# Local attention ahead of two dense layers: one TensorE product per head on 64 rows, a PSUM bank per head

## What is computed

```python
chunk, left_ctx, right_ctx = (32, 16, 8)          # B, H, S, D = 4, 8, 768, 64; 8 memory keys per head
for c in range(S // chunk):
    k_full = concat([mem_k, k[:, :, l_start:r_end]]); v_full = likewise
    scores = (q_c @ k_full.T) / 8;  a = softmax(scores);  out[:, :, c] = a @ v_full
x = out as (3072 tokens, 512)
h = x @ w_in                     # 512 -> 2048
x = (h * cos(h)) @ w_out         # 2048 -> 512
h = max(x @ w1, x @ w2, x @ w3)  # 512 -> 768
return h @ w_out2                # 768 -> 512
```

## Time and profile before

| what | us |
|---|---|
| median of 3 runs | 1005.51 |
| the three runs | 1004.49, 2384.58, 1005.51 |
| the profiled execution, its time | 1003.52 |
| its span (first to last instruction) | 1001.7 |
| TensorE matmul busy | 962.1 (96%) |
| VectorE, ScalarE, GpSimd busy | 675.9, 516.0, 210.2 |

### The profile page before, as it was taken

How to read it: one execution, slowest core, us unless ns; L and a number is a source line. 1 busy time by engine, 2 the same in 40 slices (tenths; PEclk the granted TensorE clock), 3 DMA queues, 4 the chain that set the end, 5 groups by cost and what they waited for, 6 DMA issues and landing times.

```text
span 1001.7 us, 18402 instructions
## 1 busy us (share of the span) xinstructions
PE 962.1 (96%) x7564; PEld 933.3 (93%) x7564; DVE 675.9 (67%) x926; ACT 516.0 (52%) x689; POOL 210.2 (21%) x231
## 2 busy tenths in 40 slices
PE   5989999999999999999999999999999999999998
PEld 4878889898989899989999999999999999999998
DVE  4355666566665568997998989866736546577761
ACT  1586786867778788333433334543323224444441
POOL 3341111112121212100100000662100000584610
PEclk6799999999999999999999999999999999999999
DMA  9983656574653434443445434432020031324532
GB/s 223 227 212 101 185 149 187 145 201 129 192 165 111 149 131 155 149 145 125 149 145 172 148 106 133 140 120 92 32 95 32 33 127 48 121 95 146 192 116 84
DMA packets 65395, 135.41 MB, mean 135 GB/s; under 512 B 5920, under 2 KB 27424, under 8 KB 65312
## 3 DMA queue, kind: packets, MB, share of 16 engines
q1 hardware_dynamic: 54944, 98.58, 34.2%
q0 software_dynamic: 10368, 35.66, 10.8%
HBM read 87.03 MB, written 47.19 MB: 134 GB/s over the span
## 4 chain that ended last, share of the span: by engine, by line
PE 73%; ACT 10%; DVE 9%; DMA 4%; issue 3%; POOL 1%; SPq 1%; DVEq 0%; ACTq 0%
PE ps L595 23%; PE ps L597 22%; PE ps L596 22%; PE ps L611 2%; DVE work L1178 2%; ACT work L901 2%; PE ps L636 2%; DVE units L1215 2%; ACT work L896 1%; ACT work L903 1%; PE ps L645 1%; DMA early_qk<-qk_in 1%; DVE ssum L1145 1%; ACT work L893 1%; ACT work L872 1%
## 5 line engine op out<-in xcount | busy, mean ns | idle before, releaser
L595 PE MATMUL ps<-units 128*128 128x384 f32 (+1 forms) x1940 | 611.1, 315 | 8.3 <-DVE units L1215 2.0
L597 PE MATMUL ps<-units 128*128 128x384 f32 (+1 forms) x1940 | 602.9, 311 | 0.0
L596 PE MATMUL ps<-units 128*128 128x384 f32 (+1 forms) x1940 | 602.6, 311 | 0.0
L595 PEld LDWEIGHTS ps<-units 128*128 128x128 f32 x1940 | 369.4, 190 | 20.2 <-issue 6.9
L596 PEld LDWEIGHTS ps<-units 128*128 128x128 f32 x1940 | 369.6, 191 | 0.0
L597 PEld LDWEIGHTS ps<-units 128*128 128x128 f32 x1940 | 369.2, 190 | 0.0
L921 ACT CAST units<-work 128x1024 fp32r<-128x1024 f32 x96 | 85.7, 939 | 123.9 <-DVE work L1201 106.6
L1076 ACT COPY work<-ps 128x384 f32<-128x384 f32 (+1 forms) x144 | 63.6, 454 | 146.9 <-PE ps L597 146.8
L1173 DVE SCALAR_TENSOR_TENSOR work<-work 128x768 f32<-128x768 f32 x64 | 62.2, 972 | 71.8 <-ACT work L896 71.8
L1215 DVE TENSOR_TENSOR units<-work,units 128x1024 fp32r<-128x1024 f32 x96 | 102.1, 1105 | 12.2 <-ACT units L921 12.2
L486 POOL DMA_DIRECT2D g_dram<-work x64 | 46.8, 731 | 291.4 <-DVE work L1178 286.7
(11 more groups left out here) (96 smaller groups left out, 845.4 us busy)
## 6 DMA issues: line engine op xcount, KB each, us to landing
g_dram<-work POOLq DMA_DIRECT2D x64, 384.0 KB, 3.3
work<-g_dram SPq DMA_DIRECT2D x48, 512.0 KB, 3.7
work<-qk_in SPq DMA_DIRECT2D x36, 384.0 KB, 5.3
work<-v_in SPq DMA_DIRECT2D x40, 256.0 KB, 5.0
work<-w_in POOLq DMA_DIRECT2D x40, 256.0 KB, 3.6
h_dram<-work SPq DMA_DIRECT2D x24, 384.0 KB, 2.9
work<-h_dram SPq DMA_DIRECT2D x18, 512.0 KB, 3.9
work<-y_dram SPq DMA_DIRECT2D x8, 768.0 KB, 6.5
```

Source lines behind the costliest of these rows:

```text
L595: pe.matmul(o, wh, mh, start=start, stop=False, skip_group_check=onto)
L596: pe.matmul(o, wh, ml, start=False, stop=False, skip_group_check=onto)
L597: return pe.matmul(o, wl, mh, start=False, stop=stop, skip_group_check=onto)
```

## The change

Each head gets a product of its own: stationary 64 rows by 32 columns, moving 64 rows by 64 columns, 32 products for `scores_of` and 32 for `values` in place of 16 and 16. Heads r=0 and r=1 read rows 0 to 63 and 64 to 127 and write two neighbouring banks. The zeros, their memsets and semaphores go; a subtile's keys with queries, and its values, are loaded by one DMA each. Scores (columns 0 to 255) and weighted values (columns 256 to 511) now share banks 4 and 5, turned probabilities are in 6. As two engines must not be in one bank, `values` waits for `shifted` of every scores call that stands ahead of it, and `scores_of` for `o_ready` of the values ahead of it. In block 0 `scores_of(6)` and `shift(6)` move up from f=11 to f=10. The last two pieces are of VectorE's list, block 0.

```diff
-        def scores(n):
-            return ps[:, (4, 0, 2)[n] if n < NSUB else 4, :].rearrange("p (a r k) -> p a r k", a=PAIRS, r=2)
+        def by_head(n, half):
+            if n == 1:
+                banks, at = ps[:, 0:2, :], 0
+            elif n == 2:
+                banks, at = ps[:, 2:4, :], 0
+            else:
+                banks, at = ps[:, 4:6, :], 256 * half if n else 0
+            return banks[:, :, at:at + 256].rearrange("p r (a k) -> p a r k", a=PAIRS)
+        def scores(n):
+            return by_head(n, 0)
...
         def turned(n):
-            return ps[:, (5, 1, 3)[n] if n < NSUB else 5, :].rearrange("p (a t) -> p a t", a=PAIRS)
+            return ps[:, 7 if n == 1 else 6, :].rearrange("p (a t) -> p a t", a=PAIRS)
         def weighted(n):
-            return ps[:, (4, 0, 2)[n] if n < NSUB else 6, :].rearrange("p (a r d) -> p a r d", a=PAIRS, r=2)
+            return by_head(n, 1)
...
-                for r, columns in enumerate((slice(0, KC + SUB), slice(KC, 2 * KC + SUB))):
-                    rows = slice(P // 2 * r, P // 2 * (r + 1))
-                    sp.dma_start(qk_at(n)[rows, :, columns], qk_in[n, rows, :].rearrange("p (a x) -> p a x", a=PAIRS))\
-                      .then_inc(qk_sem(n)[0], 16)
+                sp.dma_start(qk_at(n), qk_in[n, :, :].rearrange("p (a x) -> p a x", a=PAIRS)).then_inc(qk_sem(n)[0], 16)
...
-            clear_values(0)
-            clear_keys(2)
-            clear_values(1)
-            clear_values(2)
...
-            def scores_of(n):
+            def scores_of(n, values_before=0):
                 pe.wait_ge(*qk_sem(n))
-                if n < NSUB:
-                    pe.wait_ge(zeroed[n], 2)
-                else:
+                if n >= NSUB:
                     pe.wait_ge(shifted, n)
-                    pe.wait_ge(o_ready, 1)
+                    pe.wait_ge(o_ready, values_before)
                 pe.sem_inc(tiles_open, 1)
-                q = qk_at(n)
                 for a in range(PAIRS):
                     for c in range(NCH):
                         chunk = slice(CH * c, CH * c + CH)
-                        mm = pe.matmul(scores(n)[chunk, a, :, :], q[:, a, KC + CH * c:KC + CH * c + CH],
-                                       two_parts(q, a, c, KC + SUB), start=True, stop=True)
+                        for r in range(2):
+                            mm = pe.matmul(scores(n)[chunk, a, r, :], queries_in(n, a, r, c), keys_in(n, a, r, c),
+                                           start=True, stop=True)
...
-            def values(n):
+            def values(n, scores_before=0):
                 pe.wait_ge(*v_sem(n))
-                if n < NSUB:
-                    pe.wait_ge(zeroed[3 + n], 2)
-                else:
+                if n >= NSUB:
                     pe.wait_ge(o_ready, n)
+                    pe.wait_ge(shifted, scores_before)
                 pe.wait_ge(pt_copied, n + 1)
...
                 elif f == 6:
                     turn_probs(n + 2)
-                    if later:
-                        scores_of(n + NSUB)
+                    if ahead:
+                        scores_of(n + NSUB, n + 1)
                 elif f == 7:
-                    values(n + 1)
+                    values(n + 1, n + 4 if ahead else SUBS)
...
-                elif f == 9 and later:
-                    scores_of(n + NSUB + 1)
+                elif f == 9 and ahead:
+                    scores_of(n + NSUB + 1, n + 2)
                 elif f == 11:
-                    values(n + 2)
+                    values(n + 2, n + 5 if ahead else SUBS)
...
                             normalise(n + 1)
-                            shift(n + NSUB)
...
                         if f == 10:
+                            shift(n + NSUB)
                             x_low(n)
```

More of the change, by code:

```diff
@@ L104, in program @@
         LEFTOVER = 7 * UCOLS + 6 * 1024
[L105 to L106 removed]
+        early_qk = [plain(f"early_qk{i}", UCOLS * i, PAIRS * (KC + SUB)) for i in range(2)]
+        early_v = [plain(f"early_v{i}", UCOLS * (2 + i), PAIRS * KC) for i in range(2)]
         raw_rows = [plain(f"raw_wi{i}", at, 512 * n) for i, (at, n) in
@@ L314, in load_v @@
                     sp.wait_ge(pv_done, n - 2)
[L315 to L318, removed]
+                sp.dma_start(vals_at(n), v_in[n, :, :]).then_inc(v_sem(n)[0], 16)
             def load_wi(f):
@@ L635, in values @@
                         chunk = slice(CH * c, CH * c + CH)
-                        mm = pe.matmul(weighted(n)[chunk, a, :, :], prob_t(n)[:, a, chunk],
-                                       values_in(n, a, c), start=True, stop=True)
+                        for r in range(2):
+                            mm = pe.matmul(weighted(n)[chunk, a, r, :], prob_t(n)[head_rows(r), a, chunk],
+                                           values_in(n, a, r, c), start=True, stop=True)
                 mm.then_inc(pv_done, 1)
@@ L665, in attend_first @@
                 n = NSUB
[L666 to L671, removed]
+                if f in (0, 2, 4):
+                    scores_of(n + f // 2, n)
                 elif f == 7:
@@ L674, in attend_first @@
                 elif f == 9:
-                    values(n)
+                    values(n, n + 3)
                     turn_probs(n + 1)
@@ L679, in attend_first @@
                     turn_probs(n + 2)
+                    scores_of(n + NSUB, n + 1)
                 elif f == 11:
-                    values(n + 1)
-                    scores_of(n + NSUB)
+                    values(n + 1, n + 4)
                 elif f == 12:
                     turn_out(n + 1)
-                    scores_of(n + NSUB + 1)
+                    scores_of(n + NSUB + 1, n + 2)
                 elif f == 13:
-                    values(n + 2)
+                    values(n + 2, n + 5)
                 elif f == 14:
                     turn_out(n + 2)
-                    scores_of(n + NSUB + 2)
+                    scores_of(n + NSUB + 2, n + 3)
             def attend(t, f):
                 n = NSUB * (t + 1)
-                later = t < NBLK - 2
+                ahead = t < NBLK - 2
                 if f == 1:
```

49 lines of the change are left out of this document (20 added, 29 removed).

## The result

| | before | after |
|---|---|---|
| median, us | 1004.2 (8 runs) | 1011.4 (8 runs, 1008.86 to 1014.69) |
| ratio, 95% interval | | 1.0057 [1.0035, 1.0079] |
| profiled execution: time, span | 1003.52, 1001.7 | 1012.34, 1010.5 |
| TensorE matmul busy | 962.1 | 953.3 |

The change costs 0.6% by this ratio, and the medians are 7.2 us apart: no difference at 2%, but a slower kernel beyond its interval. One of the eight runs before took 2384.58 us, for which nothing here gives a reason, and the ratio leaves it out. The forecast was 1006 in a range of 998 to 1019. The sum of its terms was +1.8 us and the profiled executions differ by 8.8; the table shows that this difference hides two large misses of opposite sign.

The account below looks back on a forecast made before the run. TensorE is busy 96%, but half of each block's chain runs over ScalarE and VectorE, so only five attention groups can give time back. -2.8 - 0.8 - 1.0 + 7.2 - 0.8 = +1.8 us, forecast 1006, range 998 to 1019 with rival 2.

Parts of the forecast that it names:

- The size of a group: Attention groups on TensorE: each saves 0.40 us, within bounds of 0.43 saved and 0.8 lost.
- the supply of instructions: Within each attention group: under 7 ns an instruction, so 128 take at most 0.86 us and maybe half.
- Rival 2: Attention groups: row halves take turns, a group costs what it did, new waits stay; +13.3 us, 1017.5; chance 20%.
- Rival 3: Each of 48 groups: a floor per instruction, slower above about 0.014 us a record; +35 us, 1039; chance 8%.
- The first wait: Blocks 1 to 5, f=7: `values(n+1)` waits for `shift(n+3)`, starting 10.65 us behind `turn_out(n)` for 8.52.
- The second wait: Blocks 1 to 5, f=11: `values(n+2)` waits for `shift(n+4)`, starting 5.89 us behind the scores for 5.39.
- A block: Blocks 1 to 5, `turn_out(n)` to `turn_out(n)`: 46.9 us for 45.5, each 1.4 longer.
- +7.2: Blocks 1 to 5 together: the added waits make each 1.4 us longer, five times.
- The head: Subtiles 0 to 2: -2.8 us, from shorter groups (2.3) and one DMA for two (0.5).
- shorter groups in the head: `scores_of(2)`, `values(1)` and `values(2)` at the lower clock: 0.77 us less each, 2.3 us.
- Block 0: Block 0: -0.8 us from two scores groups ahead of the first evacuation, -1.0 from `turn_out(3)` on.
- Block 6 and the rest: Block 6 has no scores; its two values save 0.8 us, as the third waits anyway.

Follow-up runs that it names:

- E8: Changed kernel with only the first 32 of 64 keys of every score product from subtile 3 on; 1010.61 us in a single run.
- E10: Changed kernel with `sums_w1` later and both shifts earlier on VectorE, the first ahead of `gated`, the second ahead of `turn`; 995.33 us, ratio 0.9913.
- E1: Kernel before with only the new waits and the two moves in block 0, its products, banks and loads kept; 1019.64 us, ratio 1.0147.
- E4: Changed kernel with `sums_w1` moved on VectorE from f=5 to f=8, behind the first `shift` of a block; 1000.04 us, ratio 0.9944.
- E3: Changed kernel, still one DMA a subtile, but each row of keys with queries lands in four pieces of 1.5 KB; 1011.97 us, ratio 1.0061.
- E2: Changed kernel with keys with queries, and values, each loaded by two DMAs of 64 rows instead of one; 1021.81 us, ratio 1.0162.
- E7: Kernel before with only two VectorE moves, `sums_w1` behind f=8 and `shift(n+4)` ahead of `turn` at f=9; 1004.27 us, ratio 1.0004.
- E11: Same kernel as E6, measured again as the base for E10; 996.53 us, ratio 0.992.
- E5: Changed kernel with `shift(n+4)` ahead of `turn` and `gated` of f=9 on VectorE; 1009.96 us, ratio 1.0057.
- E6: Changed kernel with both VectorE moves, `sums_w1` behind f=8 and `shift(n+4)` ahead of `turn` at f=9; 996.73 us, ratio 0.9926.

## Why the forecast came out right, and where its terms did not

- **The size of a group** ("I take 0.40"): nearly twice too much, inside its bounds. It saves 1.01 - 0.79 = 0.22 us, and lasts 0.86 where "about 0.65" was to be seen. The term that failed is the supply of instructions: I had bounded it by "under 7 ns each" and then subtracted 0.03. A cost of 10 ns a record, of one load and one matmul, sets most of the pace (E8). The five groups of TensorE's half give 1.1 us a block, and E10's 44.3 for 45.5 is about that gain with the waits gone.
- **Rival 2, the row halves take turns:** false. At the lower clock `values(1)` lasts 1.18 us (17.19, above) where it lasted 1.94; its last record starts 0.86 behind its first. A wave of 64 columns takes 0.107 at this clock, half of the prediction's 0.21 for 128; sixteen of them in turn would put the last start at 1.6.
- **Rival 3, a floor per instruction:** there is one, but at 10 ns, under the 14 from which it decides. What the Trainium skill gives (TensorE: Matmul & The Clock Gate, Wait — 56ns, not 53.3ns?), 25 ns from start to start, does not hold for products on different tiles: 64 starts lie within 0.64 us.
- **The first wait** ("values(n+1) 10.65"): right in place and cause, and near in size. Measured 10.26, 10.61, 11.82, 11.27 and 10.26. The second and fourth have a memset ahead of the `shift` (0.35 us), the third had a clock drop that cost 1.6 ahead of it, and in the fourth ScalarE had waited 2.16 us for a store to DRAM, a wait that the prediction names in block 0 only. The release takes 0.21 for the 0.25 I used. E1 has it alone, E4 takes it away.
- **The second wait** ("5.89 behind the scores"): 5.86.
- **A block** ("46.9 for 45.5"): 47.7 without a clock drop (block 2), of which 0.5 are groups saving 0.22 for 0.40 (three behind the wait) and 0.36 a longer way to `turn_out` in that block alone. It is there in all nine kernels with the new products and in none of the three with the old; its cause stays open. The other four are 48.5, 48.6, 49.7 and 48.5.
- **The clock** had no term at all, and is most of what separates +7.2 from +15.4; the groups' 0.5 a block are 2.7 more. Four drops in five blocks cost some 1.5 us each, about 6: in block 1, for instance, `turn_out(n+1)` starts 4.50 us behind `values(n+1)` instead of 2.97. I had priced the idle stretch of 2.5 us as only its length. I should have asked what a new idle stretch does to the work behind it. Which drops the new waits cause is shown only in part: three of the four began close behind them and are gone in E4, but drops behind the wait for `turn_out` stay (see the last section).
- **The head** ("one DMA for two mostly saves SyncE issue time: between 0 and 1.0"): this step failed worst. The head has 4.9 us less than forecast in the table's pair, 2.8 on the mean of the traces named under E3. I read the DMA engines as full, and took full for fast: their busy share was 1.0 at half the rate. The Trainium skill has the rule, and I didn't weigh it (SBUF — State Buffer, Door 1: The DMA port swizzle (why `[64,N]` ≈ `[32,N]`)): 64 partitions that are a half of SBUF reach 8 of its 16 DMA ports, for which it gives about 218 GB/s, and 128 reach all, 436. The windows agree, with 220 to 227 and 401. The 2.3 us for shorter groups in the head are not shown by themselves: with the loads in halves (E2) the first wide matmul stands at 32.40, only 0.4 ahead of the kernel before and behind E1 and E7.
- **Block 0** ("-1.8", measured -0.7) is two misses. From the first wide matmul to `turn_out(3)` it took 34.98 us for 36.91, 1.9 less where 0.8 was forecast; the wait for the store to DRAM (9.03) is no longer in the chain. From there to `turn_out(6)` it took 1.2 more where 1.0 less was forecast. `values(4)` starts 6.19 us behind `turn_out(3)` for the forecast 4.7, with no idle time ahead of it, so not for `shift(6)`: TensorE ran at 1.2 GHz from 58.2 to 65.1, across `turn_out(3)` at 60.06, where the drop before the change (62.9 to 66.4) ended ahead of it. The four groups behind add 0.7.
- **Block 6 and the rest** ("-0.8", measured +1.8): inside block 6 the two groups do save, 0.5 us (its last `turn_out` is 20.03 us behind the first for 20.52). Over the kernels with the change this part takes 669.3 us (E3, no clock drop in it) to 673.3 (E11, two). With one drop each, six of them take 671.8 to 672.4, and the three with the old products 670.3 to 671.2, though the layers behind block 6 are untouched. Why is open.

So the total came near by luck: the head's unforeseen 4.9 us stood against the clock's 6 and the groups' missing 0.18 each. The sign was right for its reason, and the waits are shown to be that reason (E1, E4, E7).

## What to carry to other kernels

When buffers are merged so that one engine's next step waits for another engine's list, read in that list what stands ahead of the releaser, and move it in the same change: here one digit (E4) turned a loss of 0.6% into a gain of 0.6%, and two moves into one of 0.8% (three: 0.9%, not told apart). A busy DMA engine is not a fast one: read GB/s beside its share, and load all 128 rows with one transfer (E2: two transfers of 64 rows, 10 us slower). A new idle stretch on TensorE is to be priced with a possible clock drop behind it, not by its length alone.

## What the runs showed of the hardware

- Loads from DRAM to 64 rows move 220 to 227 GB/s with the DMA engines fully busy, to 128 rows 401 (E2 against the changed kernel, the same bytes and packets of about the same size).
- Products on 64 rows and 32 columns run side by side on the row halves (at 1.2 GHz the last of 64 starts 0.86 us behind the first, where sixteen waves in turn would make it 1.6). At 2.4 GHz they start about 10 ns apart with 64 moving columns and 9 ns with 32 (E8), loads of stationary data included.
- Ahead of `values(n+1)` TensorE was idle for 1.87 to 3.13 us in the 25 blocks of the kernel after the change, E2, E3, E5 and E8. In 13 of them (3 of 5 after the change) the granted clock fell to 0.50, that is 1.2 GHz, for 3.4 us (once 6.8), beginning between 1.1 us before the end of the idle stretch and 1.6 us behind it. The length does not decide it: E5 has 1.88 us with a drop and 3.13 without. In E1, with the old groups and 1.67 to 3.70 us of idle, it fell in 1 block of 5, behind the longest; in E4, E6, E10 and E11, with at most 1.08 us, in none of 20. Why E1 was spared where the changed kernel was not is open; all are one execution each.
- The wait for `turn_out(n)`, which every kernel has, is 1.75 to 2.23 us in blocks 1 to 5 of the nine kernels with the new products, and a drop began within 1.6 us of its end in 9 of 45 blocks; with the old products (before, E1, E7) it is 1.6 us, with none in 15.
- In the head of the changed kernels the 64 records of `scores_of(2)` are cut: 9 start at 11.5 us, the other 55 at 13.4, with nothing named that they wait for. E2 and E3 show the same (17.1 and 19.4, 12.4 and 14.3), the kernel before does not. No run was made on its cause.
